# Row maxima of attention scores: twelve of fifteen blocks computed as six pairs of row tiles

## The reference

```
q_pool = q.reshape(B, H, S // 2, 2, D).mean(axis=3)
scores = 1/sqrt(D) * q_pool @ k^T                    # 576 x 1152 for each head
attn   = exp(scores - max(scores)); attn /= sum(attn) + 1e-9
x      = attn @ v                                    # then the two expert layers, with routing
```

## Time and profile before

| | us |
|---|---|
| median of 3 runs (1138.81 to 1142.6) | 1141.26 |
| the profiled execution | 1139.82 |
| its span on the core | 1138.1 |
| TensorE busy | 1093.4 |
| VectorE busy | 740.7 |
| ScalarE busy | 531.8 |
| GpSimd busy | 452.8 |

### The profile page before, as it was taken

How to read it: one execution, slowest core, us unless ns; L and a number is a source line. 1 busy time by engine, 2 the same in 40 slices (tenths; PEclk the granted TensorE clock), 3 DMA queues, 4 the chain that set the end, 5 groups by cost and what they waited for, 6 DMA issues and landing times.

```text
span 1138.1 us, 22000 instructions
## 1 busy us (share of the span) xinstructions
PE 1093.4 (96%) x7757; PEld 916.7 (81%) x7757; DVE 740.7 (65%) x1706; ACT 531.8 (47%) x945; POOL 452.8 (40%) x339
## 2 busy tenths in 40 slices
PE   7999999999999999999779999999699999999996
PEld 6777777777777777777578999999589999999995
DVE  7767767887778777785436777676445655555641
ACT  3566655555655555564124444444143434353420
POOL 0768877677877788677600000000000000001000
PEclk8999999999999999999899999999799999999998
DMA  5272225223322233211649014447384281241100
GB/s 130 66 229 74 63 74 147 74 69 92 102 64 73 74 94 93 76 33 39 220 159 366 28 37 177 170 173 273 134 322 132 111 317 54 58 156 37 46 10 15
DMA packets 74397, 132.59 MB, mean 117 GB/s; under 512 B 11040, under 2 KB 29472, under 8 KB 74320
## 3 DMA queue, kind: packets, MB, share of 16 engines
q10 hardware_dynamic: 26240, 69.22, 16.8%
q1 hardware_dynamic: 43424, 50.58, 16.6%
q0 software_dynamic: 4656, 11.79, 3.0%
HBM read 106.12 MB, written 19.24 MB: 110 GB/s over the span
## 4 chain that ended last, share of the span: by engine, by line
PE 86%; DVE 5%; issue 2%; DMA 2%; POOL 2%; ACTq 1%; ACT 1%; SPq 0%; DVEq 0%; POOLq 0%
PE PS L734 20%; PE PS L587 13%; PE PS L556 9%; PE PS L504 8%; PE PS L566 7%; PE PS L571 7%; PE PS L751 6%; PE PS L747 6%; PE PS L748 6%; DVE W2L L1142 2%; PE PS L622 1%; PE PS L600 1%; PE PS L766 1%; POOL arena_a L446 1%; DMA moe<-xs 1%
## 5 line engine op out<-in xcount | busy, mean ns | idle before, releaser
L446 POOL TENSOR_TENSOR arena_a<-arena_a,arena_p 128x576 f32<-128x576 f32 x224 | 332.9, 1486 | 86.6 <-ACT arena_p L850 63.8
L1037 DVE TENSOR_REDUCE mx<-PS 128x1 f32<-128x384 f32 (+1 forms) x480 | 246.8, 551 | 110.6 <-PE PS L556 106.7
L734 PE MATMUL PS<-moe,W 128*128 128x128 f32 x2432 | 281.3, 277 | 1.6 <-ACT moe L936 1.6
L734 PEld LDWEIGHTS PS<-moe,W 128*128 128x128 f32 x2432 | 278.4, 193 | 4.0 <-ACT moe L936 2.2
L850 ACT ACTIVATE arena_p<-PS 128x576 f32<-128x576 f32 x288 | 187.7, 653 | 135.7 <-PE PS L571 135.1
L566 PE MATMUL PS<-QHT,KA 128*128 128x288 f32 x576 | 187.1, 329 | 0.0
L556 PE MATMUL PS<-KA,QHT 128*128 128x384 f32 (+1 forms) x480 | 176.1, 368 | 1.8 <-DVE mx L1037 1.8
L571 PE MATMUL PS<-QLT,KB 65*128 65x288 f32 x576 | 171.3, 301 | 0.3 <-ACT QLT L861 0.3
L822 ACT CAST W2H<-W2R 128x1024 fp32r<-128x1024 f32 x148 | 144.3, 1048 | 52.7 <-PE PS L751 39.7
L1142 DVE TENSOR_TENSOR W2L<-W2R,W2H 128x1024 fp32r<-128x1024 f32 x144 | 166.5, 1219 | 1.4 <-ACT W2H L822 1.4
L587 PE MATMUL PS<-arena_p,arena_a 128*64 128x288 f32 x1152 | 160.5, 414 | 0.0
(11 more groups left out here) (174 smaller groups left out, 1138.8 us busy)
## 6 DMA issues: line engine op xcount, KB each, us to landing
W<-in_moe_w ACTq DMA_DIRECT2D x16, 2048.0 KB, 15.0
W2R<-in_moe_w ACTq DMA_DIRECT2D x16, 2048.0 KB, 9.8
moe<-xs SPq DMA_DIRECT2D x40, 258.0 KB, 2.7
arena_a<-in_k SPq DMA_DIRECT2D x32, 288.0 KB, 2.9
arena_a<-in_v SPq DMA_DIRECT2D x32, 288.0 KB, 2.8
KB<-KA SPq DMA_DIRECT2D x32, 288.0 KB, 3.1
arena_a<-in_q SPq DMA_DIRECT2D x32, 256.0 KB, 3.2
xs<-padrow SPq DMA_DIRECT2D x8, 258.0 KB, 3.3
```

The source lines that it names most:

```text
L446: nc.gpsimd.tensor_tensor(Acc[u], Acc[u], P[u][:, t, :], ALU.add).then_inc(acc_step, 1)
L734: last = nc.tensor.matmul(PS[:, HB + f // 4, (f % 4) * PN:(f % 4 + 1) * PN], W1[s][:, d, f * PN:(f + 1) * PN], xT[:, d, :], start=(d == 0) ...
L1037: vec.reduce_max(mx3[0:n, t, c:c + 1], PS[0:n, MXB + b % 2, 0:KB_], AX.X).then_inc(pr_max, 1)
```

## The change

- The fifteen blocks become nine groups: `GROUPS` = (0), (1), (14), and the pairs (2,3), (4,5), (6,7), (8,9), (10,11), (12,13). The three single blocks are computed as before.
- A pair is two matmuls of 64 rows: the first reads rows 0 to 63 of QHT and KA (bank `MXB`), the second rows 64 to 127 of QHT and KB (bank `MXB + 1`). Both use the key high parts alone. One VectorE instruction reduces the 2 x 384 values to two columns.
- For that, KB holds the key high parts in rows 64 to 127 and ones in rows 0 to 63; QLN, QLT and the matmul at L571 have 128 rows (the negated maximum in column 0, zeros in 1 to 63, the low parts in 64 to 127). `trans_ql` transposes 128 columns and not 65.
- A pair uses both banks, so group i waits until group i - 1 is reduced; group 3 also waits for `copy_kb` of its own head.
- The steps: groups 0, 1, 2 at t = 0 (group 2 behind `trans_k`), 3 and 4 at t = 1 (before `trans_k`'s second part and behind the weighted group), 5 at t = 3, 6 and 7 at t = 4 (before and behind the last weighted group), 8 at t = 5. The weighted group 1 moves from t = 2 to t = 1. `sums` moves ahead of group 6 and the last weighted group; `back_values` and `back_sums` move ahead of group 8.
- ScalarE: `qh_out` part 1 goes ahead of the exponential of step 3, `s_out` ahead of `o_out`. VectorE: `k_low` parts 0 and 1 follow group 2, part 2 follows group 3, `q_low` follows group 6; routing steps follow groups 4 and 6.
- GpSimd zeroes both QLN tiles at the start. The pad row, zeroed at the start before, becomes part of an accumulator and is set behind the last accumulation of head 30's sums; the pad transfers wait for it.

```diff
+        GROUPS = [(0,), (1,), (NBLK - 1,), *((b, b + 1) for b in range(2, NBLK - 1, 2))]
...
-                sp.dma_start(KB[u][0:D, :].bitcast(f32), KA[g % 3][0:D, :].bitcast(f32)).then_inc(kb_in[u], 16)
+                sp.dma_start(KB[u][D:2 * D, :].bitcast(f32), KA[g % 3][0:D, :].bitcast(f32)).then_inc(kb_in[u], 16)
...
+            pool.wait_ge(sum_done, NH - 1)
+            nc.gpsimd.memset(padrow, 0.0).then_inc(pad_set, 1)
...
-                if b < 2:
+                if i < 2:
                     wait(pe, qlt_out, 2 * g)
                 else:
-                    pe.wait_ge(pr_max, NBLK * g + b - 1)
-                nc.tensor.matmul(PS[0:n, MXB + b % 2, 0:KB_], QHT[g % 3][:, t * PN:t * PN + n],
-                                 KA[g % 3][:, c * KB_:(c + 1) * KB_], start=True, stop=True).then_inc(pr_done, 1)
+                    pe.wait_ge(pr_max, NG * g + (1 if i == 2 else i))
+                if i == 3:
+                    pe.wait_ge(kb_in[g % 2], 16 * nth(g))
+                for k, b in enumerate(group):
...
+                    if len(group) == 1:
+                        last = nc.tensor.matmul(PS[0:n, MXB + i % 2, 0:KB_], QHT[g % 3][:, t * PN:t * PN + n],
+                                                KA[g % 3][:, keys], start=True, stop=True)
+                    else:
+                        rows = slice(k * D, (k + 1) * D)
+                        high = KA[g % 3] if k == 0 else KB[g % 2]
+                        last = nc.tensor.matmul(PS[0:n, MXB + k, 0:KB_], QHT[g % 3][rows, t * PN:t * PN + n],
+                                                high[rows, keys], start=True, stop=True)
+                last.then_inc(pr_done, 1)
...
+                def prior_group():
+                    if after:
+                        prior(h + 1, next(groups))
+                        if h <= 0:
+                            keep_busy(3 if h < 0 else 2)
...
+                    if t == 4 and before:
+                        sums(h - 1)
+                    if t == 5 and before:
+                        back_values(h - 1)
+                        back_sums(h - 1)
+                    if t in (0, 1, 3, 4, 5):
+                        prior_group()
...
+                if k == 1:
+                    ins = vec.reduce_max(mxf[0:n, b:b + 1], PS[0:n, MXB + i % 2, 0:KB_], AX.X)
+                else:
+                    ins = vec.reduce_max(mxf[0:n, b:b + k], PS[0:n, MXB:MXB + k, 0:KB_], AX.X)
+                ins.then_inc(pr_max, 1)
...
-                vec.tensor_reduce(QLN[g % 2][:, :, D:D + 1].bitcast(f32r), mx3[:, :, :], AX.X, ALU.max,
+                vec.tensor_reduce(QLN[g % 2][:, :, 0:1].bitcast(f32r), mx3[:, :, :], AX.X, ALU.max,
```

More of the change, by code:

```diff
@@ L108, in attention_moe_moe @@
         KA = [at(f"KA{u}", M_K + 4 * u * S, [PN, S], f32r) for u in range(3)]
-        KB = [at(f"KB{u}", M_K + 4 * (3 + u) * S, [D + 1, S], f32r) for u in range(2)]
+        KB = [at(f"KB{u}", M_K + 4 * (3 + u) * S, [PN, S], f32r) for u in range(2)]
         QHT = [at(f"QHT{u}", M_K + 4 * (5 * S + u * SQ), [PN, SQ], f32r) for u in range(3)]
-        QLT = [at(f"QLT{u}", M_K + 4 * (5 * S + (3 + u) * SQ), [D + 1, SQ], f32r) for u in range(2)]
+        QLT = [at(f"QLT{u}", M_K + 4 * (5 * S + (3 + u) * SQ), [PN, SQ], f32r) for u in range(2)]
         OT = sb("OT", [PN, HQ])
@@ L141, in attention_moe_moe @@
         moe = at("moe", M_A, [PN, (XR + 4) * ROW + 2 * DM])
-        assert (XR + 4) * ROW + 2 * DM <= A_W
+        assert (XR + 4) * ROW + 2 * DM <= A_W - 2 * SQ and NH % 2 == 0 and ROW <= SQ
         a_at = [0]
@@ L317, in pad_regions @@
         def pad_regions(eng, m, experts):
+            eng.wait_ge(pad_set, 2)
             eng.wait_ge(counts[m], 1)
@@ L432, in _ @@
             nc.gpsimd.iota(idx_i[:, :], pattern=[[OP, NT]], base=0, channel_multiplier=1).then_inc(consts, 1)
+            for u in range(2):
+                ins = nc.gpsimd.memset(view["qln"][u], 0.0)
+            ins.then_inc(consts, 1)
             def accumulate(g):
@@ L470, in _ @@
                     scatter_rows(*SCATTER_IN[h])
+            pool.wait_ge(sum_done, NH - 1)
+            nc.gpsimd.memset(padrow, 0.0).then_inc(pad_set, 1)
+            pool.wait_ge(pad_set, 1)
+            nc.gpsimd.memset(padrow[:, C_IDX:C_IDX + 1], NO_TOKEN).then_inc(pad_set, 1)
             scatter_rows(B - 1)
@@ L650, in body @@
                 now, after, before = has(h), has(h + 1), has(h - 1)
-                blocks = iter(range(NBLK))
+                groups = iter(range(NG))
+                def prior_group():
[3 more added lines that the diff above has]
+                            keep_busy(3 if h < 0 else 2)
                 for t in range(KT):
@@ L656, in body @@
                         scores(h, t, 0)
[L657 to L660, removed]
+                    if t == 0:
+                        prior_group()
                     if now:
                         scores(h, t, 1)
[L663 to L666, removed]
+                    if t == 4 and before:
[4 more added lines that the diff above has]
+                    if t in (0, 1, 3, 4, 5):
+                        prior_group()
                     if t == 0:
@@ L671, in body @@
                                 keep_busy(14)
+                        prior_group()
                         if before:
                             weighted(h - 1, 0)
[L674 to L679, removed]
+                    if t == 1:
+                        if has(h + 2):
+                            trans_k(h + 2, 1)
+                            if h == FIRST:
+                                keep_busy(5)
+                        if before:
+                            weighted(h - 1, 1)
+                        prior_group()
                     if t == 3 and has(h + 2):
@@ L890, in body @@
                             qh_out(h + 2, 0)
+                            qh_out(h + 2, 1)
                     if has(h - 1) and t == 5:
+                        s_out(h - 1)
                         o_out(h - 1)
-                        s_out(h - 1)
                     if has(h):
@@ L984, in _ @@
             for u in range(2):
-                vec.memset(KB[u][D:D + 1, :].bitcast(f32), 1.0)
+                vec.memset(KB[u][0:D, :].bitcast(f32), 1.0)
             vec.memset(mx3[:, :, :], 0.0)
@@ L1155, in body @@
                     pool_q(h + 2)
-                for b in range(NBLK):
+                for i in range(NG):
                     if has(h + 1):
-                        block_max(h + 1, b)
+                        block_max(h + 1, i)
                     if has(h + 2):
-                        if b == 1:
+                        if i == 2:
                             k_low(h + 2, 0)
                             k_low(h + 2, 1)
-                        if b == 5:
+                        if i == 3:
                             k_low(h + 2, 2)
-                        if b == 7:
+                        if i == 6:
                             q_low(h + 2)
-                    route_in(b)
+                    route_in({4: 5, 6: 9}.get(i))
                 if has(h + 1):
```

45 lines of the change are left out of this document (23 added, 22 removed).

## The result

The changed kernel takes 1186.2 us (median of 4 runs, 1183.4 to 1190.0), the kernel before 1140.8: ratio 1.040, 95% interval 1.037 to 1.042. The profiled execution has a span of 1184.9 us against 1138.1, so there are 46.8 us to account for. The forecast was 1171, range 1118 to 1184: the right sign, the time outside the range, and the loss forecast a third too small.

The account below looks back on a forecast made before the run. The prediction took TensorE's own order to bound the kernel. Steady bodies at +0.62 us a head times 30 (+18.6), late copies (+7.3) and the start (+5) made +31 on 1139.8, so 1171 us, range 1118 to 1184.

Parts of the forecast that it names:

- Item 1: Steady bodies, streaming on TensorE: six overlapped pairs replace twelve blocks, -1.08 us a head.
- Items 2 and 3: TensorE in steady bodies: nine more array switches, +0.90 us a head, and weights exposed behind switches, +0.80.
- Item 4: Pairs waiting for the previous group's reduction, single buffered: taken as 0, bound +0.3 us a head, 9 us.
- Item 5: Wider trans_ql, L571 with 128 rows, ScalarE's reordering, GpSimd's zeroing and pad row: nothing; weight-load bound 0.25 us a head.
- Item 6: Group 3's new wait for the copy into KB: two late copies cost +2.8 and +4.5, together +7.3 us.
- Item 7: The start: head 0's group 3 waits for its copy, then six pairs follow singly; +5 us, bounds +3 and +8.
- (a): Rival: pairs overlap and switching costs nothing, 1124 us, faster; chance 0.30.
- (b): Rival: pairs neither overlap nor switch, so TensorE gains nothing, 1155 us; chance 0.20 together with (c).
- (d): Rival: no overlap and the full price of switches, 1203 us; chance 0.05.
- (c): Rival: pairs overlap and pay lateness, but weights load under it, 1152 us; chance 0.20 together with (b).

Follow-up runs that it names:

- e2: Changed kernel with both matmuls of a pair in rows 0 to 63 and no wait for the copy into KB: 1204.3 us.
- e8: Changed kernel with full-row pairs, no copy wait, routing steps behind group 7 and the last head's sums behind its last weighted group: 1156.7 us.
- e1: Changed kernel with both matmuls of a pair using all 128 rows, so no row tiles and no wait for the copy into KB: 1169.4 us.
- e9: e7 with groups 3 and 5 in full rows, the copy wait at group 4 and the first 4 MB of weight loads in two bodies: 1148.4 us.
- e4: Changed kernel with the routing steps that follow group 6's reduction moved behind group 7's: 1172.4 us.
- e6: Changed kernel with the last head's row sums behind its last weighted group again: 1183.1 us.
- e3: Changed kernel with full-row pairs, but group 3 still waiting for the copy into KB: 1185.3 us.
- e5: Changed kernel with head 0's copy into KB issued ahead of SyncE's small loads of router weights: 1180.1 us.
- e7: Changed kernel with the edits of e4, e5, e6 and e10 together, row tiles kept: 1158.2 us.
- e10: Changed kernel with the two early expert weight loads issued in step 3 of the next body, behind the copy into KB: 1181.1 us.

## Why the prediction was wrong, by its own steps

- **Item 1, streaming (-1.08 a head): right.** Pairs start together, and e2, which takes the overlap away and keeps the tiles, has a steady body 1.05 longer than the changed kernel's and costs 18 us more even without the copy's waits.
- **Items 2 and 3, switches (+1.70 a head): the unit prices right, the sum too large.** A steady body grew by 0.20 and not 0.62, 6 us and not 18.6. The items' count splits in two. From the kernel before to the pairs in full rows it gives 0.20, and e8 has 0.29. From full rows to row tiles it gives +0.80 + 0.70 - 1.08 = +0.42, and the steady bodies have -0.07. So the error of 0.49 lies in the second part. By the starts of the two steady bodies of e1 and of the changed kernel it lies at two groups. The tiles cost 0.14 more at group 3 (0.17 by the count), 0.04 at groups 4 and 7 together (0.04), and save 0.17 at group 6 (0.18); but group 5 costs 0.04 and not 0.22, and group 8 saves 0.14 where 0.17 more were counted. At both TensorE's queue waits for another engine in e1: behind group 5 the next weights wait 0.22 us for a copy by ScalarE (134.45 us), and at group 8 0.23 us for the reduction of group 7 (122.81 us). There the edges lie in part inside a wait. This split is read from the starts; e9 confirms groups 3 and 5 (0.17 a body), and no run isolates group 8.
- **Item 4, single buffering (0, bound +0.3 a head): the step that failed.** 15.4 us, of which e4 gives back 13.9. I listed "q_low or routing steps" as what would push group 7's reduction, and then put the term at nothing because the switches would fill the gap. The body that I read for it has routing steps, just ahead of the reductions of the earlier trace rows:

```profile
314.03 0.53 DVE L1083 TENSOR_TENSOR gex<-L,gmx 96x96 f32<-96x96 f32 x1
314.49 0.24 DVE L1085 TENSOR_TENSOR gc<-L,gmx 96x96 f32<-96x96 f32 x1
```

They held nobody, since VectorE then waits 1.02 us for TensorE; with two banks in turns a late reduction has a block of slack, and with both banks in one group it has none. 18 bodies carry routing. Sixteen of them grew beyond the 0.20, thirteen by 0.6 to 1.1 us and the three with ranks by 1.5; of the other two one is the late copy's and one the last. In bodies without routing the term was right.
- **Item 5, what costs nothing: the last body was left out.** There TensorE waits for GpSimd in the row sums, which now stand ahead of the last weighted group: 3.1 us by e6. The other 2 us of the tail are not settled.
- **Item 6, the copy (+7.3): right mechanism, 11.5 measured.** The waits are 2.8 and 4.1, where 2.8 and 4.5 were forecast; what I did not price is TensorE's clock, half granted for 3.3 and 4.5 us behind them. About 0.8 of the 11.5 are routing steps in the second body. e3 against e1 gives 15.9 for the copies and the start together.
- **Item 7, the start (+5, bounds 3 to 8): 8.5 measured,** 5.8 at head 0 (6.1 back in e5) and 2.7 in the next body, where I had written that head 1 wins a little back. "The idle engine's clock costs a little more" was the short part: it stayed at half up to 35 us.

In numbers: 31 forecast, +15.4 for routing, -12.6 for the switches, +4.2 for the copies, +3.5 for the start, +5.4 for the tail: 46.9 against 46.8 in the profiled executions. The sum closes by construction, since the 15.4 is what the other parts leave; the check on it is e4's 13.9. That 1171 came as near as it did is luck: the switches, 12.6 too dear, hid most of the term that was put at nothing. With the steady body right the same working gives 1158. The upper end of the range, 1184, fell short because item 4's bound of 9 us was taken from the stated shortfall without the routing steps, and no bound was set for the tail.

Of the rivals, (a) is refuted by the edges in every pair, (b) and (d) by the overlap, (c) by the weights that are exposed at each edge.

## What to carry to other kernels

Before tiling the array, count the switches at both edges and the weights exposed behind each, and set them against the streaming saved. Here the overlap of six pairs gave 1.05 us a head and switching in and out cost 0.98. Groups 3 and 5, alone between ungrouped matmuls, lost 0.17 a body (e9 against e7); the other four, three of them beside a grouped matmul and group 8 behind a wait, together came out 0.25 ahead (e9 against e8). Take out of such a count the edges that lie inside a wait for another engine.

When one instruction consumes two buffers at once, double buffering is gone, and then every instruction that stands ahead of the consumer on its engine counts, in every kind of body; read the worst body and not the typical one. A step that held nobody before can hold the whole queue after.

A transfer whose first reader is moved up must be checked at its latest landing and at the start, and the clock behind the wait priced too.

## What the runs showed of the hardware

- Two 64-row fp32r matmuls in the two row halves start within 0.01 us of each other, and the pair has the same edges as the column groups: 0.09 to 0.10 late at each switch and about 0.10 for 128 columns of weights that are no longer hidden. A 64-row tile at row 0 alone pays them (e2); a block of 64 columns at column 0 does not.
- In e1, where the array is whole, the second block of a pair starts 0.28 behind the first when the pair follows the weighted group (121.14 and 121.42), 0.23 when it is group 8, of 64 columns, behind a wait (122.81 and 123.04), and 0.17 otherwise (130.04 and 130.21).
- TensorE waited 4.1 us, up to 194.1. The granted clock was half from 192.0 to 198.6, so for 4.5 us of the work behind the wait. The wait and the clock together cost this body 6.3 us (23.9 against 17.6 in e10).
- Two loads of 2 MB each, issued together at 71.6 us, and a 288 KB copy issued at 81.4 took 6.9 us to landing in e10, 3.4 for the copy at the same place in the changed kernel. A single load issued 7.4 us behind a copy (193.9 and 186.5) disturbed neither that copy nor the next: both landed after 3.0.
